# Retention, soft experts and top-2 experts on one core: SW's late rows between the products of tile 0, ranks in 16 bits, shorter tables

## The reference, cut to what matters

```
attention:  state = gamma_h * state + k_t v_t^T;  y_t = scale * q_t state      (B=4, H=8, S=768, D=64)
x = y as 3072 x 512
soft MoE:   logits = x @ phi                                                    (32 slots, 8 experts x 4)
            slot_in = softmax over tokens(logits)^T @ x
            slot_out[e] = relu(slot_in[e] @ w1[e]) @ w2[e]                      (F=1024)
            x = c @ slot_out,   c = softmax over slots(logits)
top-2 MoE:  noisy = x @ w_gate + log1p(exp(x @ w_noise)) * noise                (8 experts)
            the two largest per token, weights by softmax of the two
            out[token] += weight * (relu(x @ w1[e]) @ w2[e])                    (F=1024)
```

## Time and profile before

| | us |
|---|---|
| median of 3 runs | 548.78 (547.09, 548.78, 551.18) |
| the profiled execution | 547.3 |
| its span | 545.6 |
| PE busy | 496.7 (91%) |
| DVE / ACT / POOL busy | 277.1 / 185.3 / 257.9 |
| mean granted PE clock | 0.969 |

### The profile page before, as it was taken

How to read it: one execution, slowest core, us unless ns; L and a number is a source line. 1 busy time by engine, 2 the same in 40 slices (tenths; PEclk the granted TensorE clock), 3 DMA queues, 4 the chain that set the end, 5 groups by cost and what they waited for, 6 DMA issues and landing times.

```text
span 545.6 us, 13537 instructions
## 1 busy us (share of the span) xinstructions
PE 496.7 (91%) x4845; PEld 294.6 (54%) x4846; DVE 277.1 (51%) x449; ACT 185.3 (34%) x345; POOL 257.9 (47%) x216
## 2 busy tenths in 40 slices
PE   4898989997977568799999999999999999999995
PEld 4686777873476344345545455454554545545452
DVE  1775757565411698573564645454646242332422
ACT  0121222222000835773645544536352222322210
POOL 1222221212000016455686868686887766656543
PEclk9999999998997688899999999999999999999998
DMA  7999999988999999415554452123232343333410
GB/s 274 358 353 417 373 379 389 336 337 305 420 424 426 403 414 380 165 51 193 188 191 136 125 179 55 30 52 52 36 59 43 47 57 44 47 50 41 55 24 1
DMA packets 32358, 107.91 MB, mean 198 GB/s; under 512 B 11567, under 2 KB 12831, under 8 KB 27840
## 3 DMA queue, kind: packets, MB, share of 16 engines
q1 hardware_dynamic: 18144, 92.89, 44.0%
q0 software_dynamic: 14176, 14.49, 14.7%
HBM read 93.87 MB, written 29.43 MB: 226 GB/s over the span
## 4 chain that ended last, share of the span: by engine, by line
PE 81%; DMA 7%; DVE 6%; issue 3%; ACT 1%; POOL 1%; SPq 0%; DVEq 0%; POOLq 0%
PE ps L988 51%; PE ps L971 5%; PE ps L655 4%; PE ps L719 4%; DMA late_w1a<-chunks 3%; PE ps L861 3%; PE ps L839 3%; DMA w_region<-chunks 3%; PE ps L695 2%; PE ps L709 2%; PE ps L730 1%; PE ps L669 1%; DMA rec_region<-records,idx 1%; PE ps L751 1%; PE ps L922 1%
## 5 line engine op out<-in xcount | busy, mean ns | idle before, releaser
L988 PE MATMUL ps<-w_region,s_region 128*128 (+1 forms) x1320 | 294.9, 380 | 1.1 <-ACT s_region L1177 1.1
L988 PEld LDWEIGHTS ps<-w_region,s_region 128*128 128x128 f16 x1320 | 127.1, 98 | 144.8 <-issue 2.6
L1607 DVE SCALAR_TENSOR_TENSOR s_region<-ps,s_region 128x1024 f16<-128x1024 f32 x55 | 67.4, 1225 | 147.0 <-ACT s_region L1177 147.0
L1177 ACT ACTIVATE s_region<-ps 128x1024 f16<-128x1024 f32 x55 | 56.3, 1024 | 182.3 <-PE ps L971 182.3
L606 POOL DMA_INDIRECT out<-s_region,rec_region x41 | 55.8, 1361 | 52.7 <-DVE s_region L1636 49.9
L612 POOL DMA_INDIRECT out<-s_region,rec_region x42 | 67.9, 1616 | 15.1 <-issue 12.2
L600 POOL DMA_INDIRECT rec_region<-records,idx x55 | 62.0, 1127 | 24.8 <-issue 16.5
L546 POOL TENSOR_TENSOR s_region<-w_region,s_region 128x512 f32<-128x512 f32 x14 | 14.8, 1058 | 51.4 <-PE ps L730 26.7
L971 PEld LDWEIGHTS ps<-s_region,sw_region 128*128 (+1 forms) x440 | 29.7, 99 | 15.7 <-issue 3.0
L1636 DVE TENSOR_SCALAR s_region<-ps,rec_region,y_scale 128x512 f32<-128x512 f32 x42 | 33.8, 805 | 6.5 <-PE ps L988 4.6
L971 PE MATMUL ps<-s_region,sw_region 128*128 128x128 f16 x440 | 34.5, 222 | 1.9 <-ACT sw_region L1130 1.9
(11 more groups left out here) (248 smaller groups left out, 568.8 us busy)
## 6 DMA issues: line engine op xcount, KB each, us to landing
w_region<-moe_w SPq DMA_DIRECT2D x11, 2048.0 KB, 8.6
w_region<-moe_w SPq DMA_DIRECT2D x15, 1024.0 KB, 9.8
w_region<-chunks SPq DMA_DIRECT2D x26, 512.0 KB, 7.3
w_region<-moe_w SPq DMA_DIRECT2D x24, 512.0 KB, 17.2
s_region<-moe_w SPq DMA_DIRECT2D x4, 2048.0 KB, 15.1
sw_region<-chunks SPq DMA_DIRECT2D x12, 512.0 KB, 7.7
late_w1a<-chunks SPq DMA_DIRECT2D x8, 512.0 KB, 8.6
s_region<-moe_w SPq DMA_DIRECT2D x2, 1024.0 KB, 10.9
```

What stands on the lines that cost most here:

```text
L988: last = nc.tensor.matmul(bank[6 + r], h[:, r, f, :], w2b_parts[:, bass.ds(o, 1), part, f, :].rearrange("p e m -> p (e m)"), start=(first ...
L1177: nc.scalar.activation(h_hi[:, r, :, :].rearrange("p c t -> p (c t)").rearrange("p (a n) -> p a n", a=2), ps[:, 2 + 2 * r:4 + 2 * r, :], A ...
L1607: nc.vector.scalar_tensor_tensor(out=h_lo[:, r, :, :].rearrange("p c t -> p (c t)").rearrange("p (a n) -> p a n", a=2), in0=ps[:, 2 + 2 * ...
```

## The change

- The slots are turned in two halves of 64 columns, into banks 4 and 3, and copied by DVE and ACT. The gates' diagonal is one multiplication by a mask (`quarter`), not four copies.
- `chosen` and the two matrices of the ranks are 16-bit. `not_before` holds -1 for the tokens of a tile from the column's own on, so the running count plus the product gives the position without subtracting the counts. The number of tiles comes from an integer shift. Both choices' positions are computed by one pair of operations on 384 elements.
- The order of experts is found ahead of the index and of SW's first scales. The tile codes come from seven comparisons per tile with steps already weighted, in pieces between other DVE work.
- On PE, the index is waited for ahead of `sw_spread_parts(0)`, `sw_product(7)` stands ahead of `sw_spread_parts(3)`, and tile 0's hidden rows follow. Tile 0's first output products come in three parts (`first_rows`), with units 8 to 15 of SW between them. The banks and the keeper (ACT or DVE) of each unit are given by tables.
- Tiles 1 to 3 are written out. W2's o = 1 sums, scale, high and low parts move: on ACT behind `keep_ct(3, 1)`, on DVE between `h_low(2, 0)` and `keep_y(1)`, on POOL behind `add_rows(0)`. POOL does SW's second reduce after three fetches, not six.

The diff, cut to changed lines (eight columns of indentation taken off; declarations of the new small tiles, and the memsets on POOL, left out):

```diff
@@ -362,6 +366,9 @@
+SW_BANKS = (6, 1, 0, 7, 6, 1, 0, 6, 1, 0, 7, 1, 0, 7, 1, 0)
+SW_BY_DVE = (5, 9, 11, 13, 15)
+SW_BY_ACT = tuple(u for u in range(2 * E) if u not in SW_BY_DVE)
@@ -396,15 +403,18 @@
-    if unit < E:
-        return sw_act_kept, unit + 1
-    if unit < E + 4:
-        return sw_dve_kept, unit - E + 1
-    return sw_act_kept, unit - 3
+    if unit in SW_BY_DVE:
+        return sw_dve_kept, SW_BY_DVE.index(unit) + 1
+    return sw_act_kept, SW_BY_ACT.index(unit) + 1
-    return bank[(6, 1, 0)[unit % 3] if unit < E else (7, 1, 0)[(unit - E) % 3]]
+    return bank[SW_BANKS[unit]]
+def turned_slots(first, last):
+    return (bank[4 if first == 0 else 3][:, 0:(last - first) * SL].rearrange("p (c s) -> p c s", s=SL).unsqueeze(2)
+            .to_broadcast([P, last - first, REP, SL]))
@@ -551,12 +561,12 @@
...
-    nc.gpsimd.affine_select(out=before[:, :], in_=before[:, :], compare_op=ALU.is_ge, fill=0.0,
-                            base=-1, pattern=[[1, P]], channel_multiplier=-1).then_inc(consts_ready, 1)
+    nc.gpsimd.affine_select(out=not_before[:, :], in_=not_before[:, :], compare_op=ALU.is_ge, fill=0.0,
+                            base=0, pattern=[[-1, P]], channel_multiplier=1).then_inc(consts_ready, 1)
@@ -614,12 +624,11 @@
-    for i in range(DEPTH + 2):
+    for i in range(DEPTH - 1):
-    for i in range(DEPTH + 2, 2 * DEPTH + 3):
+    for i in range(DEPTH - 1, 2 * DEPTH + 3):
-    w2b_all_sum(EARLY)
@@ -632,6 +641,8 @@
+        if i == 0:
+            w2b_all_sum(EARLY)
@@ -870,10 +881,14 @@
-    nc.tensor.transpose(bank[4][:, 0:P], slot_out_4, ident[:, :]).then_inc(slot_out_turned, 1)
-    pe.wait_ge(slot_out_ready, 1)
+    pe.wait_ge(c_t_ready, 1)
+    for n in range(2):
+        part = slice(n * P // 2, (n + 1) * P // 2)
+        last = nc.tensor.transpose(bank[4 - n][:, 0:P // 2], slot_out_4[part, :], ident[part, part])
+    last.then_inc(slot_out_turned, 1)
+    pe.wait_ge(slot_out_ready, 2)
@@ -900,11 +915,16 @@
+        pe.wait_ge(sw_lo_ready, e + 1)
-            if unit >= 3 and unit not in (8, 9, 10):
-                pe.wait_ge(*sw_kept(unit - 3))
+            before_it = [u for u in range(unit) if SW_BANKS[u] == SW_BANKS[unit]]
+            if unit == 10:
+                pe.wait_ge(ct_ready, 2)
+            elif before_it:
+                pe.wait_ge(*sw_kept(before_it[-1]))
@@ -928,10 +948,8 @@
-    chosen = tmp[5].rearrange("p e t -> p (e t)")
-    nc.tensor.matmul(bank[0][:, 0:E * NT], before[:, :], chosen, start=True, stop=True)
-    nc.tensor.matmul(bank[0][:, 256:256 + E * NT], ones[:, :], chosen, start=True,
-                     stop=True).then_inc(ranks_done, 1)
+    nc.tensor.matmul(bank[0][:, 256:256 + E * NT], ones_h[:, :], chosen, start=True, stop=True)
+    nc.tensor.matmul(bank[0][:, 0:E * NT], not_before[:, :], chosen, start=True, stop=True).then_inc(ranks_done, 1)
@@ -940,11 +958,12 @@
-    pe.wait_ge(sw_lo_ready, 4)
+    pe.wait_ge(idx_ready, 1)
+    sw_product(7)
@@ -952,9 +971,8 @@
-    pe.wait_ge(idx_ready, 1)
+    pe.wait_ge(*sw_kept(3))
-    sw_product(7)
@@ -992,26 +1010,45 @@
+    def first_rows(part, chunks):
+        for f in chunks:
+            nc.tensor.matmul(bank[6], h_hi[:, 0, f, :], w2b_parts[:, 0, part, f, :],
+                             start=(part == 0 and f == 0), stop=False)
-    pe.wait_ge(*sw_kept(6))
+    turn_c(1, 1, 7)
-    turn_c(1, 1, 1)
-    out_b(0, 0, 0, True)
-    pe.wait_ge(ct_ready, 2)
-    for e in range(4, E):
-        pe.wait_ge(sw_lo_ready, e + 1)
-        sw_spread_parts(e)
+    pe.wait_ge(w2b_hi_ready, 2)
+    pe.wait_ge(h_hi_ready, 1)
+    first_rows(0, range(FC))
+    sw_spread_parts(4)
+    sw_spread_parts(5)
+    pe.wait_ge(w2b_lo_ready, 1)
+    first_rows(1, range(FC // 2))
+    sw_spread_parts(6)
+    sw_spread_parts(7)
+    first_rows(1, range(FC // 2, FC))
-    pe.wait_ge(*sw_kept(11))
+    pe.wait_ge(*sw_kept(14))
-    kept = pe.alloc_register("kept")
-    pe.reg_load(kept, tile_code[0:1, 1:2])
-    hidden_b(1, 1, expert_of(pe.snap(kept, min_val=0, max_val=E * E - 1)))
+    code = code_of(1)
+    hidden_b(1, 1, expert_of(code))
-    with pe.Fori(0, (RT - 3) // 2) as k:
+    hidden_b(2, 0, expert_of(code_of(2)))
+    turn_c(3, 1, 1)
+    o = order_of(code)
+    out_b(1, 1, o, True)
+    out_b(1, 1, o, False)
+    kept = pe.alloc_register("kept")
+    pe.reg_load(kept, tile_code[0:1, 2:3])
+    out_b(2, 0, order_of(pe.snap(kept, min_val=0, max_val=E * E - 1)), True)
+    pe.reg_load(kept, tile_code[0:1, 3:4])
+    hidden_b(3, 1, expert_of(pe.snap(kept, min_val=0, max_val=E * E - 1)))
+    turn_c(4, 0, 0)
+    out_b(2, 0, order_of(code_of(2)), False)
+    with pe.Fori(1, (RT - 3) // 2) as k:
@@ -1136,6 +1173,9 @@
+    act.wait_ge(slot_out_turned, 1)
+    nc.scalar.activation(slot_out_t[:, DC // 2:DC, :, :], turned_slots(DC // 2, DC),
+                         ACT.Copy).then_inc(slot_out_ready, 1)
@@ -1157,9 +1197,12 @@
-    for unit in range(4):
+    for unit in range(3):
+    sw_keep(3)
+    sw_keep(4)
+    sw_sums(7)
@@ -1179,22 +1222,26 @@
-    for unit in range(4, E):
-        sw_keep(unit)
+    sw_keep(6)
-    sw_sums(7)
+    sw_keep(7)
+    act.wait_ge(sw_scale_ready, 2)
+    for e in range(4, 6):
+        sw_high(e)
+    for e in range(6, E):
+        sw_high(e)
+    for unit in range(E, 2 * E, 2):
+        sw_keep(unit)
-    act.wait_ge(sw_scale_ready, 2)
-    for e in range(4, E):
-        sw_high(e)
-    w2b_sums(EARLY, junk)
-    for unit in range(E + 4, 2 * E):
-        sw_keep(unit)
+    stage_c(3, 1, rec_arrival(3))
+    h_high(2, 0)
+    keep_ct(3, 1)
+    w2b_sums(EARLY, junk)
@@ -1204,7 +1251,8 @@
-        stage_high(i, i % DEPTH, rec_arrival(i))
+        if i > 3:
+            stage_high(i, i % DEPTH, rec_arrival(i))
@@ -1453,18 +1502,14 @@
-    nc.vector.tensor_copy(slot_out_t[:, :, :, :],
-                          bank[4][:, 0:DC * SL].rearrange("p (c s) -> p c s", c=DC).unsqueeze(2)
-                          .to_broadcast([P, DC, REP, SL])).then_inc(slot_out_ready, 1)
+    nc.vector.tensor_copy(slot_out_t[:, 0:DC // 2, :, :], turned_slots(0, DC // 2)).then_inc(slot_out_ready, 1)
-    for n in range(REP):
-        part = slice(n * SL, (n + 1) * SL)
-        last = nc.vector.tensor_copy(g_diag[part, n, :], bank[6][part, 256:256 + 2 * E])
-    last.then_inc(g_ready, 1)
...
@@ -1482,8 +1527,10 @@
+    nc.vector.tensor_tensor(chosen.rearrange("p (e t) -> p e t", e=E), one1, one2, ALU.add).then_inc(chosen_ready, 1)
-    nc.vector.tensor_tensor(chosen, one1, one2, ALU.add).then_inc(chosen_ready, 1)
+    link(nc.vector.memset(reset, 1.0))
+    link(nc.vector.memset(reset[:, :, 0:1], 0.0))
@@ -1492,16 +1539,14 @@
-    link(nc.vector.tensor_copy(cnt, bank[0][:, 256:256 + E * NT].rearrange("p (e t) -> p e t", e=E)))
-    link(nc.vector.memset(reset, 1.0))
-    link(nc.vector.memset(reset[:, :, 0:1], 0.0))
-    link(nc.vector.tensor_tensor_scan(out=incl.rearrange(flat), data0=reset.rearrange(flat), data1=cnt.rearrange(flat),
-                                      initial=0.0, op0=ALU.mult, op1=ALU.add))
-    link(nc.vector.tensor_copy(per_e[:, 0, :], incl[:, :, NT - 1]))
-    link(nc.vector.tensor_tensor(eq, over_t(per_e[:, 0, :]), over_e(step[:, :]), ALU.is_gt))
-    link(nc.vector.tensor_reduce(per_e[:, 1, :], eq, AX_X, ALU.add))
-    link(nc.vector.tensor_scalar(per_e[:, 1, :], per_e[:, 1, :], 1.0, None, ALU.max))
+    link(nc.vector.tensor_tensor_scan(out=incl.rearrange(flat), data0=reset.rearrange(flat),
+                                      data1=bank[0][:, 256:256 + E * NT], initial=0.0, op0=ALU.mult, op1=ALU.add))
+    tiles_i = per_e[:, 0, :].bitcast(I32)
+    link(nc.vector.tensor_tensor(slots, incl, bank[0][:, 0:E * NT].rearrange("p (e t) -> p e t", e=E), ALU.add))
+    link(nc.vector.tensor_scalar(tiles_i, incl[:, :, NT - 1], float(P - 1), None, ALU.add))
+    link(nc.vector.tensor_scalar(tiles_i, tiles_i, P.bit_length() - 1, None, ALU.logical_shift_right))
+    link(nc.vector.tensor_scalar(per_e[:, 1, :], tiles_i, 1, None, ALU.max))
@@ -1510,13 +1555,13 @@
-    link(nc.vector.tensor_scalar(per_e[:, 4, :], per_e[:, 3, :], float(P), None, ALU.mult))
-    link(nc.vector.tensor_tensor(slot_no, incl, cnt, ALU.subtract))
-    link(nc.vector.tensor_tensor(slot_no, slot_no, over_t(per_e[:, 4, :]), ALU.add))
-    link(nc.vector.tensor_tensor(slot_no, slot_no, bank[0][:, 0:E * NT].rearrange("p (e t) -> p e t", e=E), ALU.add))
-    for n, one in ((0, one1), (1, one2)):
-        link(nc.vector.tensor_tensor(eq, slot_no, one, ALU.mult))
-        link(nc.vector.tensor_reduce(pos_f[:, n, :], by_tile(eq), AX_X, ALU.add))
+    link(nc.vector.scalar_tensor_tensor(out=slot_no, in0=over_t(per_e[:, 3, :]), scalar=float(P), in1=slots,
+                                        op0=ALU.mult, op1=ALU.add))
+    both = "p (n e t) -> p n e t"
+    ones_both = r_region[:, 3 * E * NT:5 * E * NT].rearrange(both, n=2, e=E)
+    slots_both = r_region[:, 0:2 * E * NT].rearrange(both, n=2, e=E)
```

(71 more changed lines are left out.)

19 lines of the change are left out of this document (13 added, 6 removed).

## The result

The changed kernel takes 556.78 us (median of 4, 555.46 to 557.37), the kernel before in the same comparison 549.56: a ratio of 1.0145 (95% interval 1.0101 to 1.0189). It is slower, as the sum had it, but by 7.2 us where the sum said 3.5, and the time lies above the range of 545.5 to 555.5; the prediction had given 22% to a time above 554.3. Of the 1.3 us beyond the range, 0.8 are the kernel before, whose median was 548.78 when the forecast was made. The profiled execution has a span of 553.8 us against 545.6, so the two traces hold a difference of 8.2 us to explain.

A forecast was written before the change was run, and what follows sets the result against it. Weight loads were taken to bound the preparation, PE the tiles from 240 us. Gain -0.7, stall +3.2 and clock +1.0 made +3.5 us: 550.8 from the profiled 547.3, put at 551.8; range 545.5 to 555.5.

The forecast's parts named there:

- The bound of the preparation: Before the tiles, weight landings hold SW's products 6 and 7: neither moves forward by more than 0.7 us.
- The early load of the second W2: Rival, SP queue at 202 to 214 us: it takes bandwidth from expert 7's weights, giving 555.2 us; 8%.
- The DVE terms of the front: Slots, gates and ranks on DVE: masked gates like a 0.23 us operation, the 384-element reduce 1.1 us.
- The stall: Tile 3: PE waits 3.2 us for `h_high(3)` and `keep_y(1)`, queued behind the second W2's work; bounds 0 to 4.5.
- the clock: PE slow at product 6, product 7 at 1.93 us, and another 1.0 us slow behind the tile 3 stall.
- product 7's end: SW's last product on PE ends at 215.6 us instead of 217.62; ends of the estimate 215.0 and 217.6.
- from there to `hidden_b(1)`: SW's late chain and tile 0: 12.6 us after product 7 ends, where it was 11.3; `hidden_b(1)` at 228.2.
- slow clock behind `hidden_b(1)`: After PE stands about 3 us in tile 3, a clock near 0.5 costs another 1.0 us (0 to 1.5).
- the second witness: DVE's path, `w2b_low` then `keep_y(1)`, ends 18.7 us after `hidden_b(1)`, separately making PE wait at tile 3.
- My sum for PE: PE's work from `hidden_b(1)`, by which tile 3's outputs could start 15.5 us after it.
- Fetches from 204.6: Sign in the preparation: the record fetches start at 204.6 us, still 2 us earlier.
- The front's gain: Slots, gates and ranks: positions at 192.8 us instead of 195.64, about 2.9 us earlier.

The follow-up runs named there:

- experiment 3: The changed kernel without the load of expert 7's W1, whose product uses expert 6's weights: 552.73 us, ratio 1.0078 to the kernel before.
- experiment 2: The kernel before with only the change's slots, gates, ranks and shorter chain to the positions, old engine orders behind them: 547.47 us, ratio 0.9999.
- experiment 1: The changed kernel with tile 4's staging ahead of the second W2's split high and low work, tile 1's rows kept at once: 551.43 us, ratio 1.0063.
- experiment 8: The kernel before with only the second W2's sums, reduce, scale, high and low parts moved to the change's places: 556.59 us, ratio 1.0180.
- experiment 12: The changed kernel with tile 4's and 5's staging ahead of the second W2's high halves, tile 1's rows kept at once, no idle products: 550.69 us, ratio 1.0027.
- experiment 6: The kernel before with only eight idle PE products ahead of product 7 and eight ahead of the waits for `hidden_b(1)`: 545.36 us, ratio 0.9959.

## Why the prediction was wrong in its size

**Right.** The bound of the preparation: product 7 was put at 213.7 and started at 213.84, waiting for its weights, and experiment 3 shows that nothing else held it. How closely it came is in part luck: in the other traces in which product 7 waits for that landing it starts anywhere from 212.83 to 216.21. The early load of the second W2 (from 200.63, landing 13.2 to 16.6 us later) did not delay it. The Trainium skill, in DMA: Bandwidth & Descriptors, section Queues, rings and completion order, says that a DMA engine takes one ring's descriptors in order and turns between rings; the trace agrees with both halves: product 7's weights came no later than in experiment 2, where the second W2 was issued 6.3 us later, and the record write on POOL's ring took 0.52 of the 0.83 MB at 194 to 196 us from the weights. The DVE terms of the front held (0.22 us for the masked gates, 1.08 for the reduce of 384 elements taken at 1.1 with its partner at 0.56). The stall was named with its cause, the second W2's work in the written order, and experiments 1 and 8 show it as the largest part; as foreseen, `h_high(3)` ended 18.2 and tile 1's rows 18.8 us after `hidden_b(1)`.

**The step that failed: the clock.** The prediction said "I take product 6 slow and product 7 at 1.93", and "another 1.0 us" for the slow clock behind the stall. Product 6 ran at full clock, 1.93 us, behind work without a gap from 198.33 to 208.4; then it stood 2.81 us, and product 7 took 3.19. `first_rows` started after 1.7 us of standing and took 3.33 us, priced at 1.8; the old kernel stood 1.15 us there and kept its clock. And behind `hidden_b(1)` the slow stretches cost 2.2 us more than in the old kernel, not 1.0. Together:

| term | predicted | measured |
|---|---|---|
| product 7's end | -2.0 | -0.6 |
| from there to `hidden_b(1)` | +1.3 | +2.5 |
| PE standing in tiles 2 to 4 | +3.2 | +4.0 |
| slow clock behind `hidden_b(1)` | +1.0 | +2.2 |
| sum | +3.5 | +8.1 of 8.2 |

The first two lines and the last term hold 3.8 of the 4.6 us that were missing. In this one execution the clock accounts for them: product 7 lost 1.3 us to it and `first_rows` 1.5, and behind `hidden_b(1)` eight products lost 1.6 and 24 lost 1.4, where the old kernel lost 1.0. The range let the clock fall at one or two of these places, and here it fell at all of them: behind the wait for weights, the one for `h_high(0)`, the one for the last keeps, and the stall.

Over many executions the clock's part is smaller and less sure. By the ratios the change costs 1.0145, without the stall at `turn_c(4)` 1.0063, without the one at `turn_c(5)` either 1.0027, and with idle products 0.9990: steps of 4.5, 2.0 and 2.0 us, of which only the first is clear of the noise. The first holds the slow stretch behind the stall. The traces agree that the clock is what the idle products change. Without them, product 7 ran slow in five of the seven traces in which PE had stood ahead of it, `first_rows`' first eight in three of four, and the products behind `hidden_b(1)` in seven of eight. With them, in six traces, none of these ran slow.

**The stall's place and size.** I let PE run up to tile 3's first products. It stopped earlier, at `turn_c(4)` between tile 2's hidden rows and its last eight products, because ACT's staging of tile 4 stands behind the same W2 work. The eight products (1.8 us) that I had counted as cover came behind the gap. ACT's part ended 17.3 us after `hidden_b(1)` (staging done 248.1), against the 17.6 of my sum. The DVE path, which I had counted as the second witness, was ready at 249.57, before PE had come to tile 3's products, and held nothing, because PE had already stopped. My sum for PE was also added up wrongly: 1.3, 12.5, 1.0 and 1.0 us are 15.8, not 15.5, so my own terms gave a stall of 2.9 us.

**Wrong without cost.** "Fetches from 204.6" and "the fetches still 2 us earlier": the first fetch started at 207.25, as before. I had priced the record write's earlier bandwidth at nothing for the products up to 4, and had overlooked that the sort stands behind product 4. It cost nothing, since the weights of products 6 and 7 came later still. The front's gain was also put too low, at 2.9 us against 4.7 measured from the slot copy on: my listed terms already make at least 3.4, and the gate logits' twelve products took 1.55 us at full clock instead of 2.82 at a granted clock of 0.50, 1.3 us more. Experiment 2 shows the front's worth on its own: 0.9999.

## What to carry to other kernels

In a stretch that waits for loads, shortening another chain moves only the waiting: look first for the last landing and for what stands behind it in each engine's order. Work that looks hidden in an engine's free time has a place in that engine's order, and a 4 us operation ahead of a 0.3 us staging stops the engine that is the bound. Price the clock at every place where the change lets TensorE newly stand, each with its own slow stretch (here 1.3 to 1.6 us), and add them up for the upper end of the range rather than take one. They are likely costs, not certain ones, for the same stop ran at full clock in other executions.

## What the runs showed of the hardware

- PE stood 1.15 us ahead of 16 products of 512 columns and ran them in 3.61 us (0.226 each, full clock); it stood 1.74 us ahead of eight and took 3.33 (0.42 each). The length of the stop alone doesn't decide: after the same 1.74 us these eight took 3.57, 3.54 and 1.89 us in experiments 1, 3 and 12.
- With six idle products in that gap, eight took 1.89 us in both traces that have them. Idle products whose results are never read kept the clock at full in all six traces that have them. They are free only inside a wait that is there anyway: in experiment 6 they pushed product 7 back by 1.9 us.
- A write of records from POOL took 62% of the DMA engines' time in the 2 us where it ran beside the weight loads (38%). Both together moved 418 GB/s, as much as the weights alone in the same 2 us of the kernel before (418).
